# Second perceptron's up-projection as seven products of half matrices, with sums of weights streamed from DRAM

## The reference

```
scores = scale * q_c @ k_c.T;  attn = softmax(scores);  x = attn @ v_c      # per chunk of 64, then [4608, 512]
h = x @ w_in;   x = relu(h)**2 @ w_out                                      # first perceptron
h = x @ w_in2;  g = where(h >= 1, h, where(h <= -1, 0, (h + 1)**2 / 4));  out = g @ w_out2   # second
```

## Time and profile before

| | us |
|---|---|
| median of 3 runs (1634.87 to 1635.79) | 1635.43 |
| the profiled execution's own time | 1635.38 |
| its span, first to last instruction | 1633.6 |
| PE busy in the span | 1622.8 |
| DVE (VectorE) busy | 862.3 |
| ACT (ScalarE) busy | 591.6 |
| POOL (GpSimd) busy | 129.5 |

### The profile page before, as it was taken

How to read it: one execution, slowest core, us unless ns; L and a number is a source line. 1 busy time by engine, 2 the same in 40 slices (tenths; PEclk the granted TensorE clock), 3 DMA queues, 4 the chain that set the end, 5 groups by cost and what they waited for, 6 DMA issues and landing times.

```text
span 1633.6 us, 24302 instructions
## 1 busy us (share of the span) xinstructions
PE 1622.8 (99%) x9294; PEld 1341.5 (82%) x9294; DVE 862.3 (53%) x1621; ACT 591.6 (36%) x1407; POOL 129.5 (8%) x138
## 2 busy tenths in 40 slices
PE   8999999999999999999999999999999999999999
PEld 6888888888888888888888888888888888888887
DVE  5788776666676677752124434444444444443433
ACT  5564444444433444443542222222222222222222
POOL 5640000000000000001750000000000000000000
PEclk9999999999999999999999999999999999999999
DMA  9532121212112121111330010101010101010000
GB/s 194 135 86 68 26 64 40 64 29 65 40 40 57 27 60 39 53 39 65 99 99 21 1 52 1 52 1 51 0 51 0 51 0 51 0 52 0 26 1 26
DMA packets 126477, 74.69 MB, mean 46 GB/s; under 512 B 115360, under 2 KB 115360, under 8 KB 124080
## 3 DMA queue, kind: packets, MB, share of 16 engines
q1 hardware_dynamic: 118576, 55.92, 12.9%
q0 software_dynamic: 5152, 16.85, 3.7%
q10 hardware_dynamic: 2656, 0.66, 0.2%
HBM read 54.53 MB, written 18.87 MB: 45 GB/s over the span
## 4 chain that ended last, share of the span: by engine, by line
PE 98%; DMA 1%; DVE 0%; POOL 0%; issue 0%; ACT 0%; SPq 0%; DVEq 0%
PE banks L460 48%; PE banks L498 24%; PE banks L502 24%; PE banks L553 1%; PE banks L565 1%; DMA stage<-in_moe_w_out_dram 0%; DMA qk_in<-in_k_dram 0%; DMA qk_in<-in_q_dram 0%; POOL w_in_split L378 0%; DVE prob_sum L962 0%; DVE score_max L936 0%; PE banks L541 0%; DVE prob_sum_inverse L988 0%; SPq L256 0%; POOL stage L365 0%
## 5 line engine op out<-in xcount | busy, mean ns | idle before, releaser
L460 PE MATMUL banks<-x_t_split,w_in_split 128*128 128x512 f32 x3444 | 824.3, 389 | 0.0
L460 PEld LDWEIGHTS banks<-x_t_split,w_in_split 128*128 128x128 f32 x3444 | 646.6, 188 | 134.0
L498 PE MATMUL banks<-hidden_split,w_out_split 128*128 128x512 f32 x1728 | 417.9, 391 | 0.0
L502 PE MATMUL banks<-w_out_split,hidden_split 128*128 128x512 f32 x1728 | 414.8, 389 | 0.0
L502 PEld LDWEIGHTS banks<-w_out_split,hidden_split 128*128 128x128 f32 x1728 | 324.6, 188 | 67.0
L498 PEld LDWEIGHTS banks<-hidden_split,w_out_split 128*128 128x128 f32 x1728 | 322.9, 188 | 67.6 <-issue 0.2
L1034 DVE SCALAR_TENSOR_TENSOR hidden_raw<-hidden_raw 128x512 f32<-128x512 f32 x144 | 99.7, 692 | 349.0 <-ACT hidden_raw L793 349.0
L784 ACT ACTIVATE banks<-banks 128x512 f32<-128x512 f32 x144 | 84.6, 587 | 376.3 <-PE banks L460 375.7
L793 ACT ACTIVATE hidden_raw<-banks 128x512 f32<-128x512 f32 x144 | 86.1, 598 | 364.9 <-PE banks L460 364.9
L1042 DVE TENSOR_TENSOR hidden_split<-banks,hidden_split 128x512 fp32r<-128x512 f32 x144 | 99.6, 691 | 222.6 <-ACT banks L789 221.5
L797 ACT CAST hidden_split<-hidden_raw 128x512 fp32r<-128x512 f32 x144 | 89.3, 620 | 214.3 <-DVE hidden_raw L1037 212.1
(11 more groups left out here) (78 smaller groups left out, 496.8 us busy)
## 6 DMA issues: line engine op xcount, KB each, us to landing
mlp_out_t<-stage SPq DMA_DIRECT2D x9, 1024.0 KB, 3.9
v_and_probs_t<-mlp_out_t SPq DMA_DIRECT2D x9, 1024.0 KB, 6.9
qk_in<-in_q_dram SPq DMA_DIRECT2D x66, 128.0 KB, 3.0
qk_in<-in_k_dram SPq DMA_DIRECT2D x66, 128.0 KB, 3.1
v_and_probs_t<-in_v_dram SPq DMA_DIRECT2D x66, 128.0 KB, 3.2
out_dram<-stage SPq DMA_DIRECT2D x8, 1024.0 KB, 5.1
stage<-in_moe_w_in_dram POOLq DMA_DIRECT2D x16, 256.0 KB, 4.5
stage<-in_moe_w_out_dram POOLq DMA_DIRECT2D x16, 256.0 KB, 4.5
```

The costliest lines, as they stand in the source:

```text
L460: last = nc.tensor.matmul(h_ps[:, bank, :], w_in[:, kt, w, cols], x_t[:, par, x, kt, :], start=(kt == 0 and w == HI and x == HI), stop=(kt ...
L498: last = nc.tensor.matmul(acc[:, j, :], w_out[:, f, w, cols], hid[:, half, x, :], start=first, stop=end)
L502: last = nc.tensor.matmul(acc[:, j, :], hid[:, half, w, cols], w_out[:, f, x, :], start=first, stop=end)
```

## The change

In tiles 10 to 17 the up-projection of two slices (i and i + 8) is taken together, as a 2 x 2 block product of w_in (columns of slice i or i + 8, rows 0 to 255 or 256 to 511) with x (the same two halves of rows, tokens 0 to 255 or 256 to 511), in the seven-product form of Strassen and Winograd. Each of the seven products is 6 products on TensorE of 256 columns: 42 of 256 columns for a pair of slices, before 24 of 512. The products lie in halves of PSUM banks 4 to 7. ScalarE copies the first to SBUF, VectorE adds the others in seven adds of 128x256, and the chain up to `hid` runs in SBUF, with one buffer `h_relu` for both slices. TensorE's order is the seven products of pair i, then `down` of both slices of pair i - 1.

Four sums of x quarters are made for each tile by VectorE, and three plain quarters of x and the four sums are split in high and low. Four sums of weight blocks for each pair are made once by GpSimd, in 16 units of half a pair: units 0 to 6 between the weight work of tile 8, unit 7 after slice 16's, the rest after it. Each unit loads its part of w_in again (two DMAs), makes four sums of 128x128, splits them, and stores them in DRAM (`w_sums_dram`). In tiles 10 to 17 GpSimd loads 1 MB of sums for each pair, two pairs ahead, into the place of half of w_in's plain columns. `qk_in`, `qk_t` and `probs` of the attention share one area, which later holds the raw weights and their sums, and then the split sums of x (`x_sums_split`) and `h_relu`; ScalarE therefore waits at the end of tile 9 until all sums are stored. The last tile's two up slices in a row are gone; `lo_last` is used in its last `down` but one. Tiles 0 to 9 keep their products. In the new ScalarE list of a pair, x quarters go in pairs 3 to 5 and the sums in pair 7; in VectorE's the sums are made in pairs 5 and 6.

```diff
+PRODUCTS = ((("quarter", 0, 0), ("quarter", 0, 0), 4, 0),
+            (("quarter", 0, 1), ("quarter", 1, 0), 5, 0),
+            (("sum", 3), ("quarter", 1, 1), 6, 0),
+            (("sum", 1), ("sum", 1), 7, 0),
+            (("sum", 2), ("sum", 2), 4, 1),
+            (("sum", 0), ("sum", 0), 5, 1),
+            (("quarter", 1, 1), ("sum", 3), 7, 1))
+NP = len(PRODUCTS)
+SUMS_IN_USE = (1, 2, 0, 3)
+QUARTERS_IN_USE = ((0, 0), (1, 0), (1, 1))
+QUARTER_STEPS = {3: 0, 4: 1, 5: 2}
...
+    w_sums_dram = nc.dram_tensor("w_in_sums_split", [SLICE_PAIRS, P, 2, 2, TILE], F32).ap()
...
+        with nc.sbuf_tensor("shared", [P, 9 * TILE], F32) as place:
+            shared = place
+        x_sums_split = sb("x_sums_split", [P, 4, 2, 2, TILE // 2], F32R)
+        h_relu = sb("hidden_relu", [P, TILE])
+        qk_in = shared[:, 0:4 * TILE].rearrange("p (a b n) -> p a b n", a=2, b=2)
...
+        w_raw = shared[:, 4 * TILE:6 * TILE].rearrange("p (slot m k n) -> p slot m k n", slot=2, m=2, k=2)
+        w_sums = shared[:, 6 * TILE:7 * TILE].rearrange("p (c n) -> p c n", c=4)
+        w_sums_split = shared[:, 7 * TILE:9 * TILE].rearrange("p (w n) -> p w n", w=2).bitcast(F32R)
+        h_sums = raw[:]
...
+        def w_sums_in(slot):
+            at = DF // 2 + slot * TILE
+            return w_in[:, 0:2, :, at:at + TILE]
...
+            def load_raw_w(u):
+                i, j = u // 2, u % 2
+                if u >= 2:
+                    pool.wait_ge(w_summed, 4 * (u - 1))
+                for m in range(2):
+                    pool.dma_start(w_raw[:, u % 2, m, :, :],
+                                   w_in_dram[1][i + m * SLICE_PAIRS][:, j::2, :]).then_inc(w_raw_loaded[u % 2], DMA)
+            def sum_w(u):
+                a = w_raw[:, u % 2, :, :, :]
+                pool.wait_ge(w_raw_loaded[u % 2], 2 * DMA * (u // 2 + 1))
+                if u > 0:
+                    pool.wait_ge(w_sums_lo, u)
+                nc.gpsimd.tensor_tensor(w_sums[:, 0, :], a[:, 1, 0, :], a[:, 1, 1, :], ALU.add).then_inc(w_summed, 1)
+                nc.gpsimd.tensor_tensor(w_sums[:, 2, :], a[:, 0, 0, :], a[:, 1, 0, :], ALU.subtract).then_inc(w_summed, 1)
+                pool.wait_ge(w_summed, 4 * u + 2)
+                nc.gpsimd.tensor_tensor(w_sums[:, 1, :], w_sums[:, 0, :], a[:, 0, 0, :], ALU.subtract).then_inc(w_summed, 1)
+                pool.wait_ge(w_summed, 4 * u + 3)
+                nc.gpsimd.tensor_tensor(w_sums[:, 3, :], a[:, 0, 1, :], w_sums[:, 1, :], ALU.subtract).then_inc(w_summed, 1)
+                pool.wait_ge(w_summed, 4 * u + 4)
+                if u > 0:
+                    pool.wait_ge(w_sums_stored, DMA * u)
+                sums = shared[:, 6 * TILE:7 * TILE]
+                nc.gpsimd.tensor_copy(w_sums_split[:, HI, :], sums).then_inc(w_sums_hi, 1)
+                pool.wait_ge(w_sums_hi, u + 1)
+                nc.gpsimd.tensor_tensor(w_sums_split[:, LO, :], sums, w_sums_split[:, HI, :].bitcast(F32),
+                                        ALU.subtract).then_inc(w_sums_lo, 1)
+                pool.wait_ge(w_sums_lo, u + 1)
+                pool.dma_start(w_sums_dram[u // 2][:, u % 2, :, :], w_sums_split.bitcast(F32)).then_inc(w_sums_stored, DMA)
+            def load_w_sums(i, slot):
+                pool.wait_ge(w_sums_stored, DMA * 2 * (i + 1))
+                pool.dma_start(w_sums_in(slot).rearrange("p j w n -> p (j w) n"),
+                               w_sums_dram[i].rearrange("p j w n -> p (j w) n")).then_inc(w_sums_loaded[slot], DMA)
+            def tile_of_pairs(t):
+                last = isinstance(t, int) and t == END - 1
+                for i in range(SLICE_PAIRS - 2 if last else SLICE_PAIRS):
+                    pool.wait_ge(product_ready, NP * (pair_number(t, i) + 1))
+                    load_w_sums((i + 2) % SLICE_PAIRS, i % 2)
...
+            pool.wait_ge(headed, NG)
+            load_raw_w(0)
+            load_raw_w(1)
             for f in range(FT + 2):
                 if f < FT:
...
                     weights_out(f - 2, 1, late_w)
                     if f < FT:
                         load_out(f, 1, late_w)
+                if f % 2 == 0 and f >= 2:
+                    sum_w(f // 2 - 1)
+                    load_raw_w(f // 2 + 1)
+            for u in range(FT // 2, UNITS):
+                sum_w(u)
+                if u + 2 < UNITS:
+                    load_raw_w(u + 2)
+            pool.wait_ge(h_ready, FT * TILES + 12)
+            load_w_sums(0, 0)
+            pool.wait_ge(h_ready, FT * (TILES + 1))
+            load_w_sums(1, 1)
+            for t in range(TILES + 1, END):
+                tile_of_pairs(t)
...
+            def pair_up(t, i, par):
+                n = pair_number(t, i)
+                first_of_all = isinstance(t, int) and (t, i) == (TILES + 1, 0)
+                if first_of_all:
+                    pe.wait_ge(raw_ready, FT * (TILES + 1))
+                else:
+                    pe.wait_ge(added, NP * n)
+                if i == 0:
+                    pe.wait_ge(quarter_hi, 3 * (t - TILES))
+                    pe.wait_ge(quarter_lo, 3 * (t - TILES))
+                pe.wait_ge(w_sums_loaded[i % 2], DMA * (SLICE_PAIRS // 2 * (t - TILES - 1) + i // 2 + 1))
+                for p, (of_w, of_x, _, _) in enumerate(PRODUCTS):
+                    if i == 0 and of_x[0] == "sum":
+                        pe.wait_ge(x_sum_lo, 4 * (t - TILES - 1) + p - 2)
+                    if p == 4:
+                        pe.wait_ge(first_copied, n + 1)
+                    elif p >= 5:
+                        pe.wait_ge(added, NP * n + p - 4)
+                    for j in range(2):
+                        for w, x in ((HI, HI), (HI, LO), (LO, HI)):
...
+                            last = nc.tensor.matmul(product(p), weights, moving, start=(j == 0 and w == HI and x == HI),
+                                                    stop=(j == 1 and w == LO))
+                    last.then_inc(product_ready, 1)
...
+            def tile_of_pairs(t, par):
+                for i in range(SLICE_PAIRS):
+                    pair_up(t, i, par)
+                    if i > 0:
+                        down(t, 2 * i - 2, 1)
+                        down(t, 2 * i - 1, 1)
+                    else:
+                        if not (isinstance(t, int) and t == TILES + 1):
+                            down(t - 1, FT - 2, 1)
+                        down(t - 1, FT - 1, 1)
...
+                    if isinstance(t, int) and t == TILES:
+                        if X_STEP <= f < X_STEP + 3:
+                            quarter_in_hi(t, par, f - X_STEP)
+                        if f == FT - 1:
+                            act.wait_ge(w_sums_stored, DMA * UNITS)
+                            for k in range(4):
+                                x_sum_in_hi(t, k)
...
+            def tile_of_pairs(t, par):
+                goes_on = not (isinstance(t, int) and t == END - 1)
+                for i in range(SLICE_PAIRS):
+                    n, s = pair_number(t, i), FT * t + 2 * i
+                    act.wait_ge(product_ready, NP * n + 1)
+                    act.wait_ge(hid_lo, s - 1)
+                    nc.scalar.copy(h_sums[:, 0, HALF:], product(0)).then_inc(first_copied, 1)
+                    if goes_on and i == SLICE_PAIRS - 1:
+                        for k in range(4):
+                            x_sum_in_hi(t, k)
+                    for half in range(2):
+                        act.wait_ge(added, NP * n + (5, 7)[half])
+                        act.wait_ge(raw_ready, s + half)
+                        nc.scalar.activation(h_relu[:], h_sums[:, half, :], ACT.Relu, bias=0.5, scale=0.5).then_inc(relu_done, 1)
+                    act.wait_ge(slice_used, s - 1)
+                    nc.scalar.copy(hid[:, 0, HI, :], h_sums[:, 0, :]).then_inc(hid_hi, 1)
+                    if goes_on and i in QUARTER_STEPS:
+                        quarter_in_hi(t, par, QUARTER_STEPS[i])
+                    if i == 0:
+                        copy_acc(t)
+                    act.wait_ge(raw_ready, s + 2)
+                    act.wait_ge(slice_used, s)
+                    nc.scalar.copy(hid[:, 1, HI, :], h_sums[:, 1, :]).then_inc(hid_hi, 1)
...
+            def sum_x(t, part):
+                done = 4 * (t - TILES)
+                if part == 0:
+                    dve.wait_ge(quarter_lo, 3 * (t + 1 - TILES))
+                    sums = ((0, quarter(x_in, 0, 1), quarter(x_in, 0, 0)), (2, quarter(x_in, 1, 1), quarter(x_in, 0, 1)))
+                else:
+                    sums = ((1, quarter(x_in, 1, 1), x_sum(0)), (3, quarter(x_in, 1, 0), x_sum(1)))
...
+            def add(out, ready, p, other):
+                dve.wait_ge(product_ready, ready)
+                nc.vector.tensor_tensor(out, product(p), other, ALU.add).then_inc(added, 1)
+            def tile_of_pairs(t, par):
+                goes_on = not (isinstance(t, int) and t == END - 1)
```

(84 more changed lines are left out.)

95 lines of the change are left out of this document (59 added, 36 removed).

## The result

The kernel after the change took 1647.4 us (median of five runs, 1644.5 to 1651.0) against 1635.6 for the kernel before on the same chip (1634.9 to 1637.3): ratio 1.0071, 95% interval 1.0053 to 1.0088. So it is slower, by 11.8 us. The profiled execution took 1648.7 us with a span of 1646.5, 12.9 more than the span before, 1633.6.

A forecast was written before the change was run, and what follows sets the result against it. TensorE, busy 99% of the span, was taken as the bound. Terms of -26.9, +5.9, +25.4 and +1.0 summed to +5.4 us on 1635.4, forecasting 1641 us, slower, range 1628 to 1666.

The forecast's parts named there:

- Term 1: Pair's up-projection on TensorE: 42 products of 256 columns replace 24 of 512, 0.42 us less a pair, -26.9 us.
- The rule of the Trainium skill: Rival on TensorE: weight loads don't overlap products on the same rows; pair 3.9 us longer, some 1890 us; chance 0.02.
- Term 2: Stalls in the pair stage, from late VectorE adds and first-product copies: +5.9 us, bounds 0 and +38.
- The stream: Loads of 1 MB of weight sums per pair on GpSimd's queue during the pair stage: covered, at no cost.
- Term 3: GpSimd making weight sums from tile 8 on delays the start of the pair stage: +25.4 us, the deciding term.
- S: GpSimd's price for one unit of weight sums with the next raw load: 7.2 us, bounds 5.6 and 8.9.
- the clock: Granted clock may fall in TensorE's idle gaps, only the last showing: +1 us, between 0 and 5.4.
- second gate: Pair stage needs all sums made and the first 1 MB landed: delay 16S - 89.8, 25.4 us.
- first gate: Late GpSimd loads delay ScalarE's casts, so TensorE idles in tile 8: delay 6S - 19.1, 24.1 us.
- block 13: GpSimd's weight work for slice 13 in tile 8, forecast to start at 823.1 + 6S.

The follow-up runs named there:

- Experiment 6: Changed kernel with sums made in tiles 2 to 7, TensorE's loop over tiles 11 to 16 written out, x quarters one pair earlier: 1615.6 us, ratio 0.9876.
- experiment 8: Experiment 6 without the loads of stored sums after the first two (results not the reference's): 1615.1 us, ratio 0.9877.
- experiment 2: Changed kernel with all 16 weight sums made by GpSimd in tiles 2 to 7: 1623.3 us, ratio 0.9923.
- experiment 3: Changed kernel with all 16 weight sums behind all weight work, instead of seven of them between it: 1671.1 us, ratio 1.0215.
- experiment 1: Changed kernel with only TensorE's loop over tiles 11 to 16 written out: 1643.1 us, ratio 1.0053.
- experiment 4: Kernel before the change with four tiles in TensorE's loop body in place of two, some 3200 instructions: 1636.8 us, ratio 1.0010.
- experiment 5: Experiment 2, TensorE's loop kept, without the loads of stored sums after the first two (results not the reference's): 1618.6 us, ratio 0.9899.

## Why the prediction was right, and where it was off

Forecast 1641 as slower; measured 1647.4, within the range, 6 above. By the steps, on the profiled spans, where the forecast was +5.4 and the measured difference is +12.9 (the four terms below give 13.8, less the 0.8 by which tile 8 began earlier):

- **Term 1, products saved.** Forecast -26.9, measured 64 x (10.88 - 10.50) = -24.3. Of the 0.04 that a pair is longer than forecast, half stands in its up products (5.04 for 5.02) and half in its down products (5.46 for 5.44). The rule of the Trainium skill against which the row stood would have given a pair 3.9 us longer; the pairs say no.
- **Term 2, stalls.** Forecast +5.9, measured +4.7: 7 x 0.42 at pair 6 (forecast 7 x 0.5), and 1.7 at the start, where pair 1 waits for the copy of its first product (forecast 1.8 and 0.6). Experiment 6 removed the seven by the move that the account names. The stream was forecast at nothing, and experiment 8 shows that, with the exception of TensorE's branch below.
- **Term 3, the sums.** Forecast +25.4 with S = 7.2, and +1 for the clock; measured +24.4. The mechanism stands: experiment 2 removes all of it, experiment 3 moves it to the second gate. The terms were off in both directions. S was 6.37: I had charged 0.29 for every wait for GpSimd's own last result, and that is right only ahead of a DMA issue (781.19 above); between two operations it costs 0.06 to 0.08. By the first gate S = 6.37 gives 6 x 6.37 - 19.1 = 19.1. The other 5.3 are on the timelines of GpSimd and ScalarE:

```profile
792.99 0.57 POOL L437 DMA_DIRECT2D shared<-in_moe_w_out_dram  x1 [1.31 <-issue]
...
865.72 0.57 POOL L437 DMA_DIRECT2D shared<-in_moe_w_out_dram  x1 [0.30 <-POOL w_out_split L448]
```

```profile
868.77 0.62 ACT L873 CAST w_out_split<-shared 128x512 fp32r<-128x512 f32 x1 [1.57 <-DMA shared<-in_moe_w_out_dram]
...
872.02 1.06 ACT L929 COPY stage<-banks 128x512 f32<-128x512 f32 x2
```

GpSimd took 89.4 us for the eleven blocks and six sums ahead of block 13 (772.32 to 861.74) where the formula gives 88.1: 1.3, of which 1.0 is one wait for nothing shown, ahead of 792.99. From the load at 865.72 TensorE goes on 7.4 later, at 873.10, where 6.0 was counted: 1.4, most of it ScalarE's two copies of the accumulator at 872.02, which I had left out. And the last stretch at half clock covers 5.5 us of work, which costs 2.7 where 1 was taken. The falls of the clock in the middle were covered, as forecast, since GpSimd set the pace: in experiment 1, the same up to here, the first of them is missing, the next idle stretch is 4.76 in place of 3.27, and TensorE goes on 114.3 us after the start of tile 8 in place of 114.2. So the idle stretches came out at 2.0 to 3.3, not 5.3.
- **Term 3, the second gate.** Forecast as the one that decides, it did not bind, but by little: the first sums were loaded from 945.9 on and had landed at 952.5, and the pair stage began at 954.65, behind TensorE's own work. In tile 9 a sum took 7.3 on the mean, not 6.37 (experiment 3 has the slow operations). S = 7.2 was right there by luck: waits counted too dear, slow operations not foreseen.
- **Not foreseen: TensorE's branch.** +9.0 in two places: 10.50 was exceeded by 2.93 and 1.52 at the first, by 2.97 and 1.58 at the second, in each the idle time and then the half clock. The diff shows why: seven products of six half-size matmuls for a pair in place of two slices of twelve take the loop body of two tiles from 1610 instructions to 2270, counted in the traces between two branches (matmuls and weight loads alone: 2 x 768 to 2 x 1056). Before, no 16 KB block of instructions is fetched from 1091 to 1468 us; after, they are fetched all through. The Trainium skill ("Runtime: NRT & Kernel Launch", Instruction fetch mechanics) gives TensorE an instruction memory of 128 KiB, 2048 instructions, refilled in blocks of 16 KiB, and says that a taken branch whose target isn't in the window held forces a fetch before execution can go on. The traces agree: 1610 and 2270 stand on either side of 2048, and experiment 4, with some 3200, has the long branch too; where between 1610 and 2270 it sets in, no run here shows. My prediction counted instructions of TensorE as time only.

The account of who delays whom was thus right, and its near hit is in part luck. Without the branch it would have been 1638 against 1641. Within term 3, the first gate's sums were 5.0 too dear (6 x 0.83), and the 1.3, 1.4 and 1.7 above, none of them foreseen, made up for most of it.

## What to carry to other kernels

Ask of work that prepares a cheaper algorithm on which engine and in which stage it stands: here the seven products were worth 24 us, and the same sums cost 24 or nothing by their place alone. When an edit lengthens a loop body, count its instructions on each engine against what that engine holds; a loop that no longer fits pays at each taken branch, for TensorE more so behind large DMAs, and what is late behind it may be a second engine's branch. Written in its best form found, the change is 21 us faster than the kernel before (ratio 0.9867), not 12 slower.

## What the runs showed of the hardware that I had not expected

- A taken branch of TensorE took 0.24 us with a body of 1610 instructions, 3.5 to 3.9 with 2270 or 3200, and 6.4 with 1 MB loads issued from another queue; about 3.5 of it was covered by instructions already issued. VectorE's next instruction behind its branch came 2.8 us late with those loads (experiment 1) and without them (experiment 8).
- In the changed kernel the granted clock was 0.5 for 3.4 us behind five idle stretches of 2.0 to 3.3 us, and for 6.8 behind the one of 5.6; behind one more, of 2.25 up to 856.4, it did not fall. In experiment 1 it did not fall behind stretches of 2.1 and 2.2, where one of 2.0 had brought it down in the changed kernel, so that near 2 us the length alone does not tell. In experiment 3, in the wait of 44.4 us, it was 0.5 from 934.8 to 979.2, so that the first products behind it ran at half pace. After idle stretches of 0.9 and 1.1 (experiment 1) and of 0.8 and 0.9 (experiment 5) it did not fall.
- GpSimd's 128x128 sums took 0.46 us or up to 1.0, its copy of 512 columns 0.61 or up to 1.15, its remainder of 512 columns 1.28 or up to 1.8. The longer ones all began while VectorE was at an operation with both inputs in SBUF, and VectorE's of that kind, usually 0.69, mostly took longer (one 3.45) when they began while GpSimd was at work (experiment 3).
